# Attention before a mixture of experts: value product by rows of the queries, every attention matmul in two halves of 64 rows, GpSimd scaling the output, the loop over batches unrolled

## What is computed

```
scores = scale * np.matmul(q, k.transpose(0, 1, 3, 2))      # 4 x 8 x 576 x 576
...
scores = scores + bias.transpose(2, 0, 1)[None, :, :, :]    # a small network of log distances
scores = scores - np.max(scores, axis=-1, keepdims=True)
attn = np.exp(scores)
attn = attn / (np.sum(attn, axis=-1, keepdims=True) + 1e-09)
return np.matmul(attn, v)
...
logits = x @ w_gate           # x: the attention's output, 2304 tokens x 512
noisy_logits = logits + np.log1p(np.exp(x @ w_noise)) * noise
# the two best experts of a token, softmax of their two logits, then
out[mask] += top2_w[mask, k, None] * (np.maximum(x[mask] @ w1[e], 0) @ w2[e])
```

## Time and profile before

| | before |
|---|---|
| median of 3 runs | 881.14 us (880.97 to 881.75) |
| profiled execution | 881.9 us, span 880.0 us |
| TensorE busy | 815.1 us (93%), 5598 matmuls; weight loads 668.2 us (76%) |
| VectorE, ScalarE, GpSimd busy | 520.8, 414.0, 365.9 us |
| score matmuls (L551) | 105.9 + 91.3 us, 320 + 320 |
| transposes (L557) | 113.7 us, 800 |
| value matmuls (L622) | 91.5 us, 640 |
| normalization on GpSimd (L1309) | 117.5 us, 160 |
| chain that ended last | TensorE 84%, DMA 5%, VectorE 4%, ScalarE 3% |

### The profile page before, as it was taken

One profiled execution on the slowest core, in us unless ns is written; L12 is line 12 of the kernel. 1 busy time (PEld: TensorE's weight loads), 2 busy tenths in 40 slices (PEclk: granted clock), 3 DMA queues, 4 the chain that ended last, 5 costly groups with the idle time before them and its releaser, 6 DMA issues.

```text
span 880.0 us, 17622 instructions
## 1 busy us (share of the span) xinstructions
PE 815.1 (93%) x5598; PEld 668.2 (76%) x5598; DVE 520.8 (59%) x1172; ACT 414.0 (47%) x856; POOL 365.9 (42%) x376
## 2 busy tenths in 40 slices
PE   4868999999999999619999999999999999999995
PEld 1327777777777777318989889899898898998983
DVE  6967888888888888595343533624435336344311
ACT  5986777777777777512322322423223233232200
POOL 2006676676667677133144232432442324322312
PEclk9998999999999999958999999999999999999998
DMA  8784333443253441617047163380461633803113
GB/s 177 215 224 133 110 99 109 121 128 112 85 170 90 116 144 54 246 39 276 2 75 237 29 157 127 60 232 19 81 230 36 148 127 60 250 3 48 14 22 39
DMA packets 51471, 102.15 MB, mean 116 GB/s; under 512 B 12704, under 2 KB 17440, under 8 KB 51424
## 3 DMA queue, kind: packets, MB, share of 16 engines
q1 hardware_dynamic: 40240, 79.85, 29.4%
q0 software_dynamic: 10320, 21.41, 13.3%
q10 hardware_dynamic: 864, 0.29, 0.2%
HBM read 70.38 MB, written 20.53 MB: 103 GB/s over the span
## 4 chain that ended last, share of the span: by engine, by line
PE 84%; DMA 5%; DVE 4%; ACT 3%; issue 2%; POOL 0%; SPq 0%; POOLq 0%; DVEq 0%; ACTq 0%
PE ps L757 26%; PE po L772 23%; PE pt L557 12%; PE ps L551 10%; PE po L622 10%; DMA slab<-work 2%; DMA out_rows<-ys,iscat 2%; ACT work L1122 2%; ACT work L1115 1%; PE po L557 1%; DVE ohlo L1008 1%; DMA w2blk<-in_w2b 1%; DVE wlo L859 1%; PE ps L534 0%; PE po L604 0%
## 5 line engine op out<-in xcount | busy, mean ns | idle before, releaser
L757 PE MATMUL ps<-xT,whi 128*128 128x320 f32 x1024 | 177.2, 310 | 0.9 <-ACT xT L1240 0.9
L1251 ACT ACTIVATE hT<-ps 128x320 fp32r<-128x320 f32 x128 | 56.0, 437 | 233.2 <-PE ps L757 213.2
L772 PE MATMUL po<-whi,hT 128*128 128x512 f32 x640 | 162.5, 398 | 0.0
L757 PEld LDWEIGHTS ps<-xT,whi 128*128 128x128 f32 x1024 | 157.2, 189 | 1.7 <-issue 1.1
L1055 DVE SCALAR_TENSOR_TENSOR hT<-ps,hT 128x320 fp32r<-128x320 f32 x128 | 62.9, 492 | 154.4 <-ACT hT L1251 134.7
L1309 POOL TENSOR_SCALAR work<-work,rcp 128x576 f32<-128x576 f32 (+1 forms) x160 | 117.5, 744 | 85.2 <-DVE rcp L855 84.8
L840 DVE CUSTOM_DVE_ANT_0 ns<-ps,slab 128x576 f32<-128x576 f32 (+1 forms) x160 | 120.3, 752 | 33.1 <-PE ps L551 26.2
L772 PEld LDWEIGHTS po<-whi,hT 128*128 128x128 f32 x640 | 118.1, 188 | 26.9
L1150 ACT ACTIVATE work<-ns,nmax 128x576 f32<-128x576 f32 (+1 forms) x160 | 123.7, 773 | 26.3 <-DVE nmax L840 26.2
L1343 POOL DMA_INDIRECT out_rows<-ys,iscat x40 | 68.2, 1704 | 135.4 <-DMA out_rows<-ys,iscat 72.2
L557 PE MATMUL pt<-cst,work 128*128 128x128 f32 (+3 forms) x800 | 113.7, 269 | 2.4 <-DVE work L871 1.1
(11 more groups left out here) (131 smaller groups left out, 1012.8 us busy)
## 6 DMA issues: line engine op xcount, KB each, us to landing
wraw<-in_mw SPq DMA_DIRECT2D x64, 512.0 KB, 11.2
slab<-work SPq DMA_DIRECT2D x36, 288.0 KB, 3.8
qraw<-in_qT SPq DMA_DIRECT2D x66, 144.0 KB, 2.8
kraw<-in_kT SPq DMA_DIRECT2D x66, 144.0 KB, 2.9
vs<-in_v SPq DMA_DIRECT2D x32, 160.0 KB, 4.0
out_rows<-zeros SPq DMA_DIRECT2D x32, 152.0 KB
x_rows<-xnat SPq DMA_DIRECT2D x8, 576.0 KB, 5.2
wrow<-w_rows,iscat POOLq DMA_INDIRECT x40
```

Source lines behind the costliest of these rows:

```text
L757: mm = nc.tensor.matmul(bank, w1s[i][pw][:, c, f * P:(f + 1) * P], xT[px][:, c, half * HB:(half + 1) * HB], start=j == 0 and c == 0, stop= ...
L772: mm = nc.tensor.matmul(po[:, (i + t) % 2, :], hT[px][:, c, t * P:(t + 1) * P], w2s[i][pw][:, c, :], start=j == 0 and c == 0, stop=j == 2 ...
L1251: nc.scalar.activation(hT[0][:, f, half * HB:(half + 1) * HB], ps[n % 4 // 2][:, n % 2, 0:HB], ACT.Relu)\
```

## The change

- **Scores.** q and k are split by GpSimd alone (`prepare`), into `qh`, `ql`, `kh`, `kl`. Partitions 0 to 63 hold the first 288 keys of k and 64 to 127 the other 288; q stands in both. `qk` takes three products (high with high, low with high, high with low), each as two matmuls over 64 rows, one per half.
- **Transposes.** `flip` turns the unnormalized exponentials in blocks of 64 rows by 128 columns, the upper 64 rows into bank 0 and the lower into bank 1, so VectorE and ScalarE each copy 320 columns of every full tile.
- **Value product.** `pv` takes 128 query columns of `PT` as weights and streams v (64 columns), with keys in two halves of 64 partitions, into two partial sums in two banks of `po`. Output rows are query rows. It is done per tile, nine matmuls, two slots behind the transposes.
- **Scaling.** VectorE and ScalarE copy the two sums of a head (`ocopy`), GpSimd adds them and multiplies by the reciprocals (`combine`), straight into the rows of tokens `xnat`. `norm`, `oevac`, `xtile` and `xevac` are gone. For the last tile VectorE does this itself.
- **Router.** Two heads' output at a time is flipped back (`chunk`), half by half, for the logits.
- **Order.** All 160 slots are written out on every engine; SyncE's loads and stores are placed anew. The table load that was asked for ahead of the softplus is gone, and the early index searches stand later in VectorE's program.

```diff
-LAG = 5
-VLAG = NU + LAG + 1
-PVAT = {0: (0, 1, 2), 2: (3, 4)}
+LT, LV = 3, 5
+PR, ER = 4, 5
...
+            def qk(t):
+                n, u = divmod(t, NU)
...
+                for i, (qq, kk) in enumerate(((qh, kh), (ql, kh), (qh, kl))):
+                    for half in range(2):
+                        mm = nc.tensor.matmul(ps[t % 2][:, half, 0:HALF], qq[n % 2][part(half), u * P:(u + 1) * P],
+                                              kk[n % 2][part(half), :], start=i == 0, stop=i == 2)
...
+            def flip(t):
...
+                for kt in range(NU):
+                    for half in range(2 if u < NU - 1 else 1):
+                        bank = half if u < NU - 1 else n % 2
+                        mm = nc.tensor.transpose(pt[bank][:, kt * D:(kt + 1) * D], E[t % ER][part(half), kt * P:(kt + 1) * P],
+                                                 ident[part(half), part(half)])
...
+            def pv(t, dst):
+                n, u = divmod(t, NU)
+                if u == 0:
+                    pe.wait_ge(v_loaded[n % 4], 16 * (n // 4 + 1))
+                    if n:
+                        for i in range(2):
+                            pe.wait_ge(o_done[i], n)
...
+                for kt in range(NU):
+                    for half in range(2 if kt < NU - 1 else 1):
+                        mm = nc.tensor.matmul(dst[half], PT[t % PR][part(half), kt, 0:P], vs[n % 4][part(half), kt, :],
+                                              start=kt == 0, stop=kt == NU - 1 - half)
...
-                    mm = nc.tensor.matmul(po[half * D:(half + 1) * D, h % 2, 0:HALF], vs[h % 4][:, kt, :],
-                                          PT[h % 2][:, kt, half * HALF:(half + 1) * HALF],
-                                          start=kt == 0, stop=kt == NU - 1)
...
+            for t in range(TILES):
+                qk(t)
+                for x in VSLOTS.get(t, []):
+                    pv(x, partial(x % NU))
+                if t - 1 in GATE:
+                    gate(GATE[t - 1])
+                if t >= LT:
+                    flip(t - LT)
+                    if chunk_with(t - LT):
+                        chunk(*chunk_with(t - LT))
...
-                nc.gpsimd.tensor_scalar(E[i][0:r, :], E[i][0:r, :], rcp[0:r, i:i + 1], 1.0, ALU.mult, ALU.mult)\
-                    .then_inc(norm_done, 1)
...
+            def combine(n):
...
+                nc.gpsimd.tensor_tensor(osum[0][i][:, :], osum[0][i][:, :], osum[1][i][:, :], ALU.add).then_inc(sum_done, 1)
...
-            pool.wait_ge(bst_moved[2], 16 * ((GROUPS - 2 + NB - 1) // NB))
+            prepare(0)
+            prepare(1)
             pool.wait_ge(bev_done, GROUPS)
...
+            nc.gpsimd.memset(epads, 0.0).then_inc(pt_zeroed, 1)
+            for n in range(1, B * H + 1):
+                if n >= 2:
+                    combine(n - 2)
+                if n + 1 < B * H:
+                    prepare(n + 1)
```

More of the change, by code:

```diff
@@ L118 @@
-PER = [len(o) for o in ORDER]
-EARLY = [sum(before for _, before in o) for o in ORDER]
-def granule(bank, e, b, kind):
-    at = [x for x, _ in ORDER[bank]].index(e)
-    early = sum(before for _, before in ORDER[bank][:at])
-    if kind == "first":
-        return at - early
-    return b * PER[bank] - EARLY[bank] + (at if kind == "loop" else early)
-def issued(bank, h, k, now, kind, batch):
-    body = batch + (h * NU + min(k, NU - 1) + LAG >= SLOTS)
-    if body == 0:
-        return granule(bank, ("p", h, k), now, kind) + 1
-    return granule(bank, ("p", h, k), now - 1, "loop") + 1
@@ L150, in build, with uses @@
+ORDER = [bank_order(i) for i in range(2)]
+def uses(bank, e):
+    return ORDER[bank].index(e)
 def build(nc, qT, kT, v, rtab, pcol, rcp8, w1c, b1c, w2b, wg, noise, mw1, mw2, consts, out, xs):
@@ new lines, in flip_x, with chunk @@
+            def flip_x(c, half, tiles, dst):
+                b, j = divmod(c, H // 2)
+                for u in tiles:
+                    mm = nc.tensor.transpose(dst[:, u * D:(u + 1) * D], xnat[b % 2][part(half), u, j * P:(j + 1) * P],
+                                             ident[part(half), part(half)])
+                return mm
+            def chunk(c, half):
+                b, j = divmod(c, H // 2)
+                pe.wait_ge(x_done, 2 * c + 2)
+                pe.wait_ge(t_done[half], uses(half, ("x", c, half)))
+                flip_x(c, half, range(NU - half), pt[half]).then_inc(t_ready[half], 1)
@@ new lines, in partial, with logits @@
+            def partial(u):
+                return [po[:, half, u * D:(u + 1) * D] for half in range(2)]
+            def logits(chunks, halves, dst):
+                for j in chunks:
+                    for half in halves:
+                        at = 32 * (half * 2 + j % 2)
+                        mm = nc.tensor.matmul(dst[at:at + 32, 0:HALF], wgc[:, j, :], xc[:, j, half * HALF:(half + 1) * HALF],
+                                              start=j < 2, stop=j >= 2)
+                return mm
@@ new lines, in gate @@
+            def gate(b):
+                c = (b + 1) * H // 2 - 1
+                for half in range(2):
+                    pe.wait_ge(t_done[half], uses(half, ("x", c, half)) + 1)
+                pe.wait_ge(o_done[0], H * (b + 1) + 3)
+                logits(range(H // 2), range(2), po[:, 0, :]).then_inc(g_ready, 1)
+            pe.wait_ge(pt_zeroed, 2)
+            for t in range(TILES):
+                qk(t)
[7 more added lines that the diff above has]
+                        chunk(*chunk_with(t - LT))
@@ L711, in _ @@
+            logits([H // 2 - 1], range(2), po[:, 1, :]).then_inc(g_ready, 1)
+            pe.wait_ge(g_done, B)
+            folded(range(CL, NT // 2), 1)
             pe.wait_ge(r_rank, 1)
@@ L889, in _ @@
-            klow(0, 0)
-            batch(0, "first")
-            with dve.Fori(1, B) as b:
-                batch(b, "loop")
+            for t in range(TILES):
+                if t >= LT + 1:
+                    x = t - LT - 1
+                    if 0 in banks(x):
+                        evac0(x)
+                    elif chunk_with(x):
+                        evac_x(chunk_with(x)[0], NU)
+                ttr(t)
+                if t >= NU + 2 and t % NU == 2:
+                    recip((t - NU - 2) // NU)
+                if t >= NU + LV - 1 and t % NU == NU - 1:
+                    ocopy((t - NU - LV + 1) // NU)
+                if t - 1 in GATE:
+                    b = GATE[t - 1]
+                    dve.wait_ge(g_ready, b + 1)
+                    nc.vector.tensor_copy(lacc[:, b * HALF:(b + 1) * HALF], po[:, 0, 0:HALF]).then_inc(g_done, 1)
@@ L1205, in _, with evac1 @@
-            khigh(0, 0)
-            batch(0, "first")
-            with act.Fori(1, B) as b:
-                batch(b, "loop")
+            def evac1(t):
+                u = t % NU
+                at = D if u < NU - 1 else 0
+                act.wait_ge(t_ready[1], uses(1, ("p", t)) + 1)
+                if t >= PR:
+                    for half in range(2):
+                        act.wait_ge(pv_done[half], t - PR + 1)
+                nc.scalar.activation(PT[t % PR][:, :, at:at + D], pt[1][:, 0:NU * D].rearrange("p (k s) -> p k s", k=NU),
+                                     ACT.Copy).then_inc(t_done[1], 1)
```

661 lines of the change are left out of this document (281 added, 380 removed).

## The result

Four executions of the changed kernel took 895.08, 899.99, 991.02 and 993.76 us; in the last two the granted clock, averaged over the program, was 0.87 instead of 0.97 to 0.98, and the ratio leaves them out. The ratio to the kernel before is 1.018 (interval 1.012 to 1.023), so the change is **slower by 1.8%** where the clock holds; the two long executions, taken by themselves, are slower by over 12%. A second series on another occasion gave 898.32 to 905.62 us against 883.05: 1.023 (1.021 to 1.025). The profiled execution (895.08 us, span 893.2) is at the fast end of the two series.

The account below looks back on a forecast made before the run. The prediction took TensorE to bound the kernel. To the profiled 881.9 us it added 12.5 up to the last value product and 2 behind it, 896.4, less 0.8: 896 us, slower by 1.6%, range 872 to 945.

## What to carry to other kernels

Count weight loads as a resource of their own: a full-precision product loads twice, 128 weight columns cost 0.112 us each time, and streaming less than that time past them saves nothing. Alternate the row halves matmul by matmul, and keep one shape for all that stands between two waits. If loads are the bound and the clock falls, try to stream more columns past them: it cost 0 to 0.04 us a tile, and here it went with 842 us every time instead of 856 to 890. And run a kernel often enough to see whether its clock holds: the executions with and without the fall are 90 us apart here, which is more than the whole effect of the change.

## What the runs showed of the hardware

- Weight loads run with the granted clock: 0.112 us per pair of 128-column loads at 1.00, 0.213 at 0.50.
- The clock can stay at its lower level for 190 us under work that keeps TensorE's record busy throughout, and falls in 4 of 4, 5 of 11 and 0 of 5 executions of the same program with 32, 64 and 128 columns of v streamed at a time.
- Two row halves overlap where their instructions alternate (pairs 0.112 us apart); with ten of one half ahead of eight of the other, four pairs overlapped at the seam and the tile took 2.13 instead of 1.83 us.
- Loads for transposes have shorter records than loads for products of the same 64x128 (145 and 187 ns), and their pairs start 0.062 apart, not 0.112.
- A load in reduced precision is no faster than one in full precision: the value matmuls of one row half, with one instruction each, still start 0.112 apart (130.068, 130.180, 130.291).
